# Weight homes half a 128-byte line away from the feature homes, in a fused attention and two-MLP kernel on one core

## What is computed

```python
for t in range(S):
    state = f[:, :, t, :, None] * state + np.einsum('bhd,bhe->bhde', k[:, :, t], v[:, :, t])
    y[:, :, t] = np.einsum('bhd,bhde->bhe', q[:, :, t], state)      # f = sigmoid(f_logit)
x = y.transpose(0, 2, 1, 3).reshape(3072, 384)
h = x @ w_in                                                        # 384 -> 2048
x = (h * np.tanh(np.log1p(np.exp(h)))) @ w_out                      # 2048 -> 384
out = (sigmoid(x @ w_gate) * (x @ w_val)) @ w_out2                  # 384 -> 1536 -> 384
```

## Time and profile before

| | |
|---|---|
| median of 3 executions | 1032.58 us (1029.32 to 1032.74) |
| profiled execution | 1031.78 us |
| its span, first to last instruction | 1029.4 us |
| mean granted TensorE clock | 0.996 of full |
| TensorE matmul busy | 995.9 us, 97% |
| weight loads busy | 821.0 us, 80% |
| VectorE, ScalarE busy | 535.3 us (52%), 511.9 us (50%) |
| GpSimd busy | 134.0 us, 13% |
| DMA | 37.54 MB, mean 36 GB/s |

### The profile page before, as it was taken

One profiled execution on the slowest core, in us unless ns is written; L12 is line 12 of the kernel. 1 busy time (PEld: TensorE's weight loads), 2 busy tenths in 40 slices (PEclk: granted clock), 3 DMA queues, 4 the chain that ended last, 5 costly groups with the idle time before them and its releaser, 6 DMA issues.

```text
span 1029.4 us, 14241 instructions
## 1 busy us (share of the span) xinstructions
PE 995.9 (97%) x4917; PEld 821.0 (80%) x4917; DVE 535.3 (52%) x753; ACT 511.9 (50%) x865; POOL 134.0 (13%) x146
## 2 busy tenths in 40 slices
PE   3999999999999999999999899999999999999997
PEld 3988988788878888778887788888888888888885
DVE  7999995766667666687777422222222222222221
ACT  3666666777787777787777311211321122221112
POOL 2232233200000000034444500000000000000000
PEclk9999999999999999999999999999999999999999
DMA  4556541100000000001111100000100000000001
GB/s 142 166 154 176 152 139 40 39 1 1 0 1 0 0 0 0 0 24 48 53 46 47 39 1 0 1 1 1 62 0 0 0 0 25 37 0 1 1 1 62
DMA packets 35338, 37.54 MB, mean 36 GB/s; under 512 B 4064, under 2 KB 26080, under 8 KB 35296
## 3 DMA queue, kind: packets, MB, share of 16 engines
q1 hardware_dynamic: 35296, 36.98, 12.0%
HBM read 32.24 MB, written 4.72 MB: 36 GB/s over the span
## 4 chain that ended last, share of the span: by engine, by line
PE 88%; DVE 7%; issue 3%; ACT 2%; DVEq 0%; DMA 0%; ACTq 0%; SPq 0%
PE banks L820 27%; PE banks L822 27%; PE banks L821 26%; PE banks L844 2%; PE banks L859 2%; DVE suffix L644 2%; DVE prefix L661 1%; PE banks L864 1%; PE banks L876 1%; DVE xlo L694 1%; PE banks L849 0%; DVE xlo L785 0%; PE banks L886 0%; DVE probs L678 0%; PE banks L871 0%
## 5 line engine op out<-in xcount | busy, mean ns | idle before, releaser
L820 PE MATMUL banks<-xhi,whi 128*128 (+1 forms) x720 | 285.3, 396 | 2.6 <-DVE xlo L785 2.6
L822 PE MATMUL banks<-xhi,wlo 128*128 (+1 forms) x720 | 283.4, 394 | 0.0
L821 PE MATMUL banks<-xlo,whi 128*128 (+1 forms) x720 | 281.1, 390 | 0.0
L820 PE MATMUL banks<-ghi,whi 128*128 128x512 f32 x504 | 199.8, 396 | 5.4 <-DVE glo L634 5.0
L805 DVE TENSOR_TENSOR prod<-prod,banks 128x512 f32<-128x512 f32 x72 | 49.5, 687 | 292.1 <-PE banks L822 292.1
L822 PE MATMUL banks<-ghi,wlo 128*128 128x512 f32 x504 | 197.7, 392 | 0.0
L821 PE MATMUL banks<-glo,whi 128*128 128x512 f32 x504 | 196.3, 390 | 0.0
L822 PEld LDWEIGHTS banks<-xhi,wlo 128*128 128x128 f32 x720 | 135.4, 188 | 32.3
L820 PEld LDWEIGHTS banks<-xhi,whi 128*128 128x128 f32 x720 | 135.5, 188 | 31.8 <-DVE xlo L785 3.0
L821 PEld LDWEIGHTS banks<-xlo,whi 128*128 128x128 f32 x720 | 135.7, 188 | 30.9
L564 ACT ACTIVATE prod<-banks 128x512 f32<-128x512 f32 x72 | 43.1, 598 | 189.6 <-PE banks L822 189.6
(11 more groups left out here) (70 smaller groups left out, 953.4 us busy)
## 6 DMA issues: line engine op xcount, KB each, us to landing
raw<-w_out_dram SPq DMA_DIRECT2D x28, 192.0 KB, 2.4
xb<-f_dram SPq DMA_DIRECT2D x48, 96.0 KB, 2.5
kb<-k_dram SPq DMA_DIRECT2D x48, 96.0 KB, 2.3
qb<-q_dram SPq DMA_DIRECT2D x48, 96.0 KB, 2.2
vb<-v_dram SPq DMA_DIRECT2D x24, 192.0 KB, 2.4
out_dram<-rows_out SPq DMA_DIRECT2D x18, 256.0 KB, 2.1
raw<-w_in_dram SPq DMA_DIRECT2D x16, 192.0 KB, 2.7
raw<-w_gate_dram SPq DMA_DIRECT2D x12, 192.0 KB, 2.4
```

The source lines that it names most:

```text
L820: pe.matmul(ps, hi, xh, start=first, stop=False)
L821: pe.matmul(ps, hi, xl, start=False, stop=False)
L822: return pe.matmul(ps, lo, xh, start=False, stop=last)
```

## The change

`base` becomes the next multiple of 128 plus 64, and 64 bytes are left out between `wlo` and `xhi`. Instructions, their order, tiles and waits stay as they are; only the addresses differ.

```diff
+LINE, HALF_LINE = 128, 64
...
-        base = (nc.sbuf_base + 63) // 64 * 64
+        base = (nc.sbuf_base + 127) // 128 * 128 + HALF_LINE
...
         whi = sb("whi", [P, SLOTS, DM], F32R)
         wlo = sb("wlo", [P, SLOTS, DM], F32R)
+        top[0] += LINE - HALF_LINE
         xhi = sb("xhi", [P, KC, N_TOK], F32R)
```

## The result

| | before | changed |
|---|---|---|
| median of 20 runs each | 1032.53 us | 1033.97 us |
| ratio of the changed kernel to before, 95% interval | | 1.0023 (1.0012 to 1.0033) |
| profiled execution | 1031.78 us | 1035.83 us |
| its span | 1029.4 us | 1033.3 us |
| first matmul of the first MLP starts at | 161.58 us | 162.66 us |

The change costs 0.2%, some 2.4 us by the ratio. It is inside what I called no change, and it is clear of the measurement's own uncertainty.

The account below looks back on a forecast made before the run. TensorE's matmuls, covering 97% of the span, were taken to bound the kernel. Terms of -2.4 + 0 + 2.4 + 0.3 = +0.3 us, added to the profiled 1031.78 us, gave 1032.1 us, range 1024.5 to 1038.5 us.

Parts of the forecast that it names:

- Group 3: project, and project2 of blocks 0 to 9, from -64 to -128, taken as distance 0: +2.4 and +0.3 us.
- Group 1: The 96 hidden units of the first MLP go from distance 0 to -64 at project's pace: -2.4 us.
- group 2: gate and value units of blocks 0 to 10, from 0 to -64 at project's pace: -1.3 and +1.3, together 0.
- Where the time is decided: From 161 us on, the time is the number of matmuls times their start-to-start spacing; no size given.
- First and second reading: In MLP matmuls, distance counts, not place; +64 (2.10 us) and -64 (2.06) differ, so a pattern is longer than 128 bytes.
- Third reading: In the MLPs, a unit inherits the state ahead; distance 0 needs nine matmuls to settle; gate 2.08, value 2.04 us.
- Term 4, block 11: block 11, and project2 of blocks 10 and 11, in the second MLP: distances unchanged, 0 us.
- Attention stage: Ahead of the MLPs, some buffers move by 64 against the rest: taken as 0, with 1 us either way.
- Rival A: hidden, gate and value units go like block 11: +5.5 us, 1037.3 us, or +11.7 and 1043.5; chance 0.27.
- Rival B: Projections at distance 128 go at 2.04 us, the two reads meeting least: -6.7, 1025.1 us; chance 0.17.
- rival C: Homes in the MLPs do nothing; spacing differences come from unit order and waits: 1031.8 us; chance 0.11.
- The rule that I set against the forecast: For MLP matmuls, a single gap of about 216 ns and independent read ports: homes do nothing, sum 0.

Follow-up runs that it names:

- the series: Pads gave all units of the kernel before one equal distance (0, ±32, -64, ±128, ±192 or 256 bytes): ratios from 0.9881 to 1.0103.
- the kernel with 256: Pads put all weights at distance 256 bytes from their moving operands, against the kernel before: 1019.18 us, ratio 0.9881.

## Why the prediction was wrong, point by point

Two terms of the sum failed. Group 3 took distance 128 for distance 0, and its units took 2.09 to 2.10 us where I had put 2.085: +3.8 us measured, +2.7 expected. Group 1, with gate in group 2, let units at -64 run at 2.06 us although they are entered from units at -128, and they took 2.065 to 2.079: -1.2 and -0.8 us measured, -2.4 and -1.3 expected.

- **Where the time is decided** (spacing of matmuls, nothing else): right. Waits, loads' records and order are the same, and kernels that differ only in pads have medians from 1019 to 1043 us.
- **First and second reading** (distance and not place; +64 is not -64): right, and shown by everything moved by 64 (1.0004) and by the series. The row that I took for the first couldn't show it: project2 of block 10 and gate both took 2.08 us, but neither had settled. The pattern is 256 bytes as far as the distances tried tell.
- **Third reading** (a unit inherits its state, distance 0 has 2.04 as its own pace): right, and shown by distance 0 everywhere, and by hidden's 2.064 us when only its neighbours moved. It lacked that a change of place between two units at distance 0 unsettles the pace as well.
- **Term 1, hidden**: expected -2.4, measured -1.2 us. I let hidden run at 2.06 from its first matmul. Entered from a project unit at -128 it takes 2.065 to 2.079 us; entered from one at -64, in the change with its projections left at -64, it took 2.060. I had applied the third reading to group 3 and not to groups 1 and 2.
- **Term 2, gate and value**: gate expected -1.3, measured -0.8, for the same reason; value expected +1.3, measured +1.1.
- **Term 3, the projections at -128**: this is the step that failed most in its reason. I took 128 to be 0, a pattern of 128 bytes, two paragraphs after reading from the rows that the pattern must be longer. That 128 is not 0 is shown by -128 everywhere (2.10 us) beside 0 everywhere (2.04). The number was near all the same by luck, expected +2.7, measured +2.9 + 0.9 = +3.8, because I had borrowed hidden's 2.085, which is the pace of a unit at 0 that has not settled. The true price of -128 is 2.09 to 2.10 us, the upper end that I gave.
- **Term 4, block 11**: 2.10 us before and after, right.
- **Attention stage**: 1 us either way was right in size; its 1.1 us are within what two executions of one layout differ by. The upper end of my range adds up to 1037.3 + 1 = 1038.3 us, not 1038.5.

The sum in the MLPs was thus +2.9 instead of +0.3 us, all of it from terms 1 to 3. It was wrong in size by 2.6 us, a quarter of a per cent. With the 0.8 us by which I had started below the median, that also made the sign wrong. Rival A (features' units like block 11) didn't come: value went to 2.06, not 2.10. In its reason it is half alive, since -64 can run at 2.10 too, as one pass did. Rival B (128 the best) is refuted, and rival C as well: padding alone moved the time from 0.988 to 1.010 of the kernel before, and no unit went below 2.04 us, 227 ns a matmul. The rule that I set against the forecast I had also read too simply. The Trainium skill, page "TensorE: Matmul & The Clock Gate", section "Back-to-back issue gap", gives 216 ns for 512 columns as the gap of an isolated matmul, and 131 ns for a stream of weight loads and matmuls. No fp32r stream of this case went at either: the lowest was 227 ns.

What stays open: which of the two reads waits for the other and how, why the pace depends on the units before, why one distance can have two paces, and why ±32 are as slow as +64. Since -64 can go at 2.06 or 2.10 us, a distance seen only at 2.10 may have a faster pace that none of these runs fell into: ±32 were run six times each and -192 four times, and no execution came below 1040 us. These runs show that the pace hangs on the two addresses; that it is a collision of the two reads is the reading that fits, and it was not measured by itself.

## What to carry to other kernels

When TensorE is full, look at the start-to-start spacing of its matmuls, unit by unit, and compare kinds of units that do the same work; a spread of some per cent points at something that no busy time and no wait shows. Here the cure was to give weights and moving operands homes at the same residue within 256 bytes, in every stage and also in the spill-over homes: two pads, 12 us, 0.988 of the kernel before; only the kernel with 256 did as well. Changing the distance of one kind of unit alone also moves its neighbours, since a stream takes its state from the matmuls ahead: 4.5 us lost in the projections came with 3.8 us won beside them.

## What the runs showed of the hardware that I had not expected

- For fp32r matmuls of 128x128 weights and 512 columns the spacing at a granted clock of 1.00 was 227 ns (2.04 us for nine) with weights and moving operand at the same address within 256 bytes, 229 ns at -64, and 232 to 233 ns at ±32, +64 (block 11, and -192 everywhere) and ±128.
- The same instructions at the same addresses can run on at two paces (-64: 2.06 or 2.10 us a unit), for nearly a whole pass of some 150 us.
- Two neighbouring units can both have distance 0 and still lose time where the place changes between them: 2.04 us, then 2.08, with all homes of the second 64 bytes further on.
- Moving the operands of one kind of unit changed the time of its neighbours: hidden 2.086 to 2.064 us, with no change to its own homes.
